# Regrouping the transfers of the last, short tile: by token range instead of by channel block

## The reference

```python
    s = kn.transpose(0, 2, 1) @ qn / tau
    a = np.exp(s - s.max(-1, keepdims=True))
    a /= a.sum(-1, keepdims=True) + 1e-09
    x = v @ a                                  # 6016 x 256
    rms = np.sqrt(np.mean(x * x, axis=-1, keepdims=True) + 1e-06)
    xn = x / rms * rms_g
    g = xn @ w_gate                            # 256 -> 1536
    x = (g * sigmoid(g) * (xn @ w_val)) @ w_out
    h = x @ w_in                               # 256 -> 2048
    return (h - np.tanh(h)) @ w_out2
```

## Time and profile before

| | before |
|---|---|
| time, median of 3 runs | 1174.14 us (1174.03 to 1174.22) |
| the profiled execution's own time | 1174.13 us |
| its span, first to last instruction | 1172.1 us |
| PE busy | 1166.8 us |
| DVE busy | 851.9 us |
| ACT busy | 365.2 us |
| granted TensorE clock | 1.00 |

### The profile page before, as it was taken

The page is one execution under the profiler, slowest core; times in us unless marked ns, Lnnn a source line. Parts: engine busy times, 40 slices in busy tenths (PEclk is TensorE's granted clock), DMA queues, the critical chain, the costliest instruction groups (busy, mean ns, idle before and its releaser), DMA issues.

```text
span 1172.1 us, 15843 instructions
## 1 busy us (share of the span) xinstructions
PE 1166.8 (100%) x5296; PEld 979.6 (84%) x5296; DVE 851.9 (73%) x1445; ACT 365.2 (31%) x589; POOL 34.8 (3%) x26
## 2 busy tenths in 40 slices
PE   9999999999999999999999999999999999999998
PEld 8888888888888888888888888888888888888998
DVE  6888775865866767677586586676767758658666
ACT  7856512321411421321232141142132223123121
POOL 4600000000000000000000000000000000000000
PEclk9999999999999999999999999999999999999999
DMA  9613220010011001002001001100100100100100
GB/s 371 212 54 94 51 36 1 0 31 5 0 18 18 0 6 30 0 0 36 0 0 32 4 0 18 18 0 7 29 0 0 31 0 0 19 1 1 19 1 14
DMA packets 104922, 33.91 MB, mean 29 GB/s; under 512 B 92352, under 2 KB 100288, under 8 KB 104896
## 3 DMA queue, kind: packets, MB, share of 16 engines
q1 hardware_dynamic: 103008, 32.98, 11.1%
q10 hardware_dynamic: 1888, 0.59, 0.2%
HBM read 27.40 MB, written 6.16 MB: 29 GB/s over the span
## 4 chain that ended last, share of the span: by engine, by line
PE 99%; DMA 1%; SPq 0%; DVE 0%; issue 0%; ACT 0%; DVEq 0%
PE ring L1027 51%; PE out_acc L1061 22%; PE y_acc L1061 16%; PE ring L1043 3%; PE out_acc L1011 2%; PE y_acc L964 2%; PE y_acc L973 1%; DMA qk_in<-in_q_dram 1%; SPq L350 0%; PE y_acc L1027 0%; PE y_acc L1203 0%; PE out_acc L1203 0%; PE y_acc L1079 0%; PE ring L984 0%; PE y_acc L1207 0%; PE y_acc L1083 0%
## 5 line engine op out<-in xcount | busy, mean ns | idle before, releaser
L546 ACT ACTIVATE act<-ring 128x512 f32<-128x512 f32 (+1 forms) x333 | 196.3, 590 | 706.9 <-PE ring L1027 605.3
L836 DVE TENSOR_TENSOR h_lo<-act,h_hi 128x512 fp32r<-128x512 f32 (+1 forms) x336 | 228.5, 680 | 10.9
L823 DVE TENSOR_TENSOR act<-ring,act 128x512 f32<-128x512 f32 (+1 forms) x141 | 94.9, 673 | 143.4 <-ACT act L546 143.4
L832 DVE TENSOR_TENSOR act<-ring,act 128x512 f32<-128x512 f32 (+1 forms) x192 | 129.0, 672 | 76.8 <-ACT act L546 76.4
L1061 PE MATMUL out_acc<-h_hi,wl_hi 128*128 128x512 f32 (+1 forms) x384 | 147.8, 385 | 0.0
L1061 PE MATMUL out_acc<-h_hi,wl_lo 128*128 128x512 f32 (+1 forms) x384 | 147.7, 385 | 0.0
L1061 PE MATMUL out_acc<-h_lo,wl_hi 128*128 128x512 f32 (+1 forms) x384 | 147.6, 384 | 0.0
L928 DVE CAST h_hi<-act 128x512 fp32r<-128x512 f32 (+1 forms) x308 | 129.7, 421 | 12.9
L1027 PE MATMUL ring<-y_hi,wl_hi 128*128 128x512 f32 (+1 forms) x356 | 137.0, 385 | 0.0
L1027 PE MATMUL ring<-y_lo,wl_hi 128*128 128x512 f32 (+1 forms) x356 | 137.0, 385 | 0.0
L1027 PE MATMUL ring<-y_hi,wl_lo 128*128 128x512 f32 (+1 forms) x356 | 137.0, 385 | 0.0
(11 more groups left out here) (188 smaller groups left out, 1653.1 us busy)
## 6 DMA issues: line engine op xcount, KB each, us to landing
out_dram<-out_rows SPq DMA_DIRECT2D x88, 64.0 KB, 1.8
qk_in<-in_k_dram SPq DMA_DIRECT2D x9, 512.0 KB, 8.7
qk_in<-in_q_dram SPq DMA_DIRECT2D x9, 512.0 KB, 9.8
v_in<-in_v_dram SPq DMA_DIRECT2D x72, 64.0 KB, 2.2
w_in<-in_moe_w_out_dram SPq DMA_DIRECT2D x14, 256.0 KB, 3.0
w_in<-in_moe_w_in_dram SPq DMA_DIRECT2D x8, 256.0 KB, 3.3
w_in<-in_moe_w_gate_dram SPq DMA_DIRECT2D x6, 256.0 KB, 4.2
w_in<-in_moe_w_val_dram SPq DMA_DIRECT2D x6, 256.0 KB, 4.6
```

The costliest lines, as they stand in the source:

```text
L546: nc.scalar.activation(act[:, u % RING, 0:width], bank(t, name)[:, 0:width], func).then_inc(act_ready, 1)
L823: nc.vector.tensor_tensor(buf, bank(t, gate)[:, 0:width], buf, ALU.mult).then_inc(bank_free, 1)
L832: nc.vector.tensor_tensor(buf, bank(t, hidden)[:, 0:width], buf, ALU.subtract).then_inc(bank_free, 1)
L836: nc.vector.tensor_tensor(h_lo[:, u % RING, 0:width], act[:, u % RING, 0:width], f32(h_hi[:, u % RING, 0:width]), ALU.subtract).then_inc(h ...
```

## The change

The last tile, and only that, is moved in other pieces. Instead of cutting a half (128 channels) by its four blocks of channels, the new function `last_tokens` cuts it by tokens: `LAST_PARTS` = 2 parts of 192 tokens, with all four blocks of channels of the half in one transfer. The last tile of v then comes in four transfers instead of eight (two halves, two parts), all from SyncE's queue (`load_last`). For each half of the output SyncE issues part 0 and ScalarE part 1: two transfers instead of four. The bytes, the 128-byte pieces and the queue of each share are as before; the waits' constants follow the number of transfers.

Within a part, partition `q*32 + r` now holds the six successive tokens 6r to 6r+5 rather than every 32nd one. The load and the store use the same order.

```diff
+LAST_PARTS = 2
...
+    PART_BLOCKS = SHORT // SQ // LAST_PARTS
+    assert PART_BLOCKS * SQ * LAST_PARTS == SHORT
...
+    def last_tokens(rows, part, half):
+        begin = (TILES - 1) * TILE + part * PART_BLOCKS * SQ
+        return rows[begin:begin + PART_BLOCKS * SQ, half * P:(half + 1) * P].rearrange("n (q c) -> q n c", c=SQ)
...
+            def load_last():
+                for half in range(KC):
+                    for part in range(LAST_PARTS):
+                        sp.dma_start(v_in[:, half, part * PART_BLOCKS:(part + 1) * PART_BLOCKS, :],
+                                     last_tokens(v_rows, part, half)).then_inc(v_loaded, 16)
...
-                    shared = isinstance(t, int) and t == TILES - 1
-                    for quad in range(QUADS // 2 if shared else QUADS):
+                    for quad in range(QUADS):
...
-            load_v(TILES - 1, SHORT)
+            load_last()
             store(TILES - 3, TILE)
             store(TILES - 2, TILE)
-            store(TILES - 1, SHORT)
-            sp.wait_ge(stored, TILE_DMAS * TILES - TILE_DMAS // 2)
-            sp.wait_ge(stored_last, TILE_DMAS // 2)
+            for half in range(KC):
+                sp.wait_ge(out_turned, (TILES - 1) * KC + half + 1)
+                sp.dma_start(last_tokens(out, 0, half), out_rows[:, half, 0:PART_BLOCKS, :]).then_inc(stored, 16)
+            sp.wait_ge(stored, TILE_DMAS * (TILES - 1) + 16 * KC)
+            sp.wait_ge(stored_last, 16 * KC)
...
             for half in range(KC):
                 act_e.wait_ge(out_turned, (TILES - 1) * KC + half + 1)
-                for quad in range(QUADS // 2, QUADS):
-                    act_e.dma_start(tokens(out, TILES - 1, SHORT, half, quad),
-                                    out_rows[quad * SQ:(quad + 1) * SQ, half, 0:SHORT // SQ, :]).then_inc(stored_last, 16)
+                act_e.dma_start(last_tokens(out, 1, half),
+                                out_rows[:, half, PART_BLOCKS:2 * PART_BLOCKS, :]).then_inc(stored_last, 16)
...
-                dve.wait_ge(v_loaded, (t - 1) * TILE_DMAS)
+                if isinstance(t, int) and t == TILES - 1:
+                    dve.wait_ge(v_loaded, (t - 2) * TILE_DMAS + 16 * KC * LAST_PARTS)
+                else:
+                    dve.wait_ge(v_loaded, (t - 1) * TILE_DMAS)
```

## The result

| | before | changed |
|---|---|---|
| time, median | 1174.18 us (6 runs, 1173.93 to 1174.73) | 1181.63 us (6 runs, 1181.34 to 1181.96) |
| ratio | | 1.0063, 95% interval 1.0052 to 1.0074 |
| the profiled execution's own time | 1174.13 us | 1181.70 us |
| its span | 1172.1 us | 1179.9 us |
| PE busy | 1166.8 us | 1167.3 us |

The change costs 7.45 us, where 6.07 were forecast: 1181.6 instead of 1180.2, inside the range. The page of the changed kernel shows the same work on every engine; what is new lies outside it.

A forecast was written before the change was run, and what follows sets the result against it. PE bounds the kernel until its last product, then the uncovered last store does. Span 1172.1 + 6.07 (data phase 8.41 instead of 2.34) = 1178.2, plus 2.03 outside the span: 1180.2 us; range 1177.0 to 1184.0.

The forecast's parts named there:

- The number of engines: Last tile's new transfers: extents 4 and 128 allow four DMA engines instead of 16, 772 packets on each.
- the share of the DMA engines: Sign at the kernel's end: DMA share near 0.25 to 0.3, against 1.14 before.
- time to landing: Sign for the last store: about 5 us for the first half and 8 for the second, against 2.0 and 2.2.
- Both queues on the same four: Last store: SyncE's and ScalarE's transfers share the same four engines; data phase 8.41 us in place of 2.34.
- the rival with eight engines in two groups of four: Last store: each queue uses a different four, 386 packets an engine, +1.9 us, 1176.0 us; chance 0.03.
- The rivals that would have spared the time: Last store: all 16 engines, 1173.9 us, chance 0.11; or four with a quick packet, 1175.7 us at 5.0 ns, chance 0.02.
- The load: Load of tile 11, in mid-kernel: 8.4 to 16.2 us on four engines, hidden by PE's products, costed at nothing.
- The upper bound of 21 ns: Highest packet price, from the earlier load of tile 11; the store would then take 16.2 us, +13.9.
- The start stays at 1168.73: Last store: first bytes move at the same time as before, 0.84 us after the issue.
- The packet's price: Last store: 10.9 ns for each 128-byte packet on an engine, 8.41 us for 772 packets.
- the 1.03 us behind the last byte: Kernel's end: last completion returns and SyncE finishes; forecast to stay at 1.03 us.
- PE's and DVE's last instructions at the same times to 0.1 us: Sign at the kernel's end: both engines finish as before, to 0.1 us.

The follow-up runs named there:

- the series of 384, 8, 4 and 2: The changed kernel's four 96 KB stores with outermost DRAM extent 384, 8, 4 (the change itself) or 2 (load too): 1174.74, 1176.87, 1181.63 and 1190.44 us.
- The wide transfers of 96 KB: The changed kernel with its four stores patterned with 384 tokens outermost in DRAM, so on sixteen engines: 1174.74 us.

## Why the prediction was right

**The number of engines: right, and shown.** The step was a choice, since all the rows had outermost extents of 32 or 128. The count of completion packets (16 for four transfers) and the series of 384, 8, 4 and 2 settle it: the transfer ran on as many engines as the two outermost extents allow in equal shares, and the time follows the busiest engine. Two of the prediction's signs were off for four engines: the share of the DMA engines is 0.35 to 0.41 and not 0.25 to 0.3, and for the narrow transfers the profile gives no time to landing at all.

**Both queues on the same four: right.** One queue gives the same time; the rival with eight engines in two groups of four is out. What eight engines really cost (1176.87 in another shape) is 0.9 above the 1176.0 worked out for it.

**The rivals that would have spared the time: out.** Joining small transfers brought nothing by itself: with 16 engines the four large transfers measure as the eight smaller ones do. The Trainium skill's advice to join transfers (DMA: Bandwidth & Descriptors, Rules for kernel authors) does hold one size further down, where 24 KB cost 1.2 us over 48 KB; it can't be followed at the price of the engines. The Trainium skill's rule on how many engines a transfer gets (the same page, Why a DMA increments its semaphore by 16 and not by 1) agrees with every packet count here: 64, 32, 16 and 8 left-over packets for four transfers with extents of 384, 8, 4 and 2.

**The load: right.** Hidden, as the run with it alone shows. It was faster than either bound, 7.4 us instead of 8.4 to 16.2: one queue kept four engines at 54 GB/s, 9.5 ns a packet. The upper bound of 21 ns was a limit of the issue and not of the engine, as the text had suspected.

**The size: 1.4 us short.** Three terms were mis-sized, all small. *"The start stays at 1168.73"* failed: the first byte came 1.20 us after its issue instead of 0.84 (+0.36). The wide transfers of 96 KB show the same (issue at 1168.18, first byte at 1169.5), so it isn't the four engines. Nor is it the 96 KB: in the run with contiguous runs of 768 bytes, four transfers of 96 KB in 128 pieces each, the first byte came 0.86 us after the issue. It goes with the 768 pieces, where 384 and fewer took 0.82 to 0.86; why, isn't shown. The prediction had named these 768 pieces and put them at nothing, by the length of the issue instructions. The packet's price was 11.5 ns in the mean and not 10.9: 8.9 us instead of 8.41 (+0.5), made up of a slow start, a stretch at 9.5 ns and a later one at 11.7. That the forecast's 10.9 lies so near is in part luck: it was not the engines' limit, as the 9.5 ns show, and the slow stretches happen to make up for the fast one. And the 1.03 us behind the last byte became 1.25 (+0.22). That is 1.1 of the 1.4; the other 0.3 us isn't explained, and is no more than executions of one kernel differ by (1173.93 to 1174.73 before). The sign *"PE's and DVE's last instructions at the same times to 0.1 us"* was set too tight: they were 0.65 us later, with no wait added, and one execution of the same work can differ from another by that much.

Still open is why the rate of a narrow store falls after some 2 to 3 us, from 54 to 44 GB/s. The load on the same four engines keeps 54 for its whole 7 us, and in the kernel with eight engines the store falls as well, from 108 to 87 GB/s. TensorE's clock, its idleness and the second queue are excluded; nothing else was tried. One hint is in the counts: by the fall each engine had passed some 190 packets in the kernel with one queue, 200 with eight engines, 240 with two and 250 in the changed kernel. The stores on 16 engines give each engine 200 packets or fewer in all, so they may end before a fall could show; but the load passed 772 an engine without one.

The slow start is open too. In the changed kernel ScalarE's queue had moved 3 packets by 1171.1, 2.5 us after its issue began, and the rate was 21 to 49 GB/s until then; the kernel with one queue was at 53 GB/s some 0.4 us after its first byte.

No version here beats the kernel before in its own task. With 128-byte pieces on 16 engines the end is near a balance, by an estimate from the earlier trace rows: the first half's 100 packets on each engine last from 1168.73 to about 1169.82, and the second half, issued at 1168.94, can move from 1169.78.

## What to carry to other kernels

Before joining transfers, look at the outermost extent on both sides: the largest divisor up to 16 that the two share sets how many DMA engines work, and the time is that of the busiest one's packets. Halving the number of transfers was worth nothing at 48 KB, and the shape that it needed cost nearly four times the data phase; the same shape in a load that has 85 us of slack costs nothing, which is why such an edit has to be judged place by place. In a profile, the packets left over after the data pieces, divided by the number of transfers, give the engines of each, where all transfers have the same shape.

## What the runs showed that was not expected

A narrow transfer holds up what is issued behind it, wide or narrow: the next issue took 1.31 or 1.40 us on SyncE and 2.75 on ScalarE, against 0.32 to 0.52; and of two narrow issues begun together on two queues one took 0.60 and the other 1.43. A store of 768 pieces moved its first byte 1.2 to 1.4 us after its issue, one of 128 to 384 pieces after 0.82 to 0.86, whether it had 24, 48 or 96 KB. And on eight, four or two engines a store of 128-byte pieces slows from 9.5 to 11.7 ns a packet after 2 to 3 us, while a load of the same pieces on four engines doesn't.
